# One program per engine for recurrence, branch and dense part; the guard in front of the last product; the second product three tiles behind

## The reference

```python
for t in range(S):
    y[:, :, t] = np.einsum('bhd,bhde->bhe', rt, state)
    Sa = np.einsum('bhde,bhe->bhd', state, at)
    state_decay = state * wt[:, :, None, :] - np.einsum('bhd,bhe->bhde', Sa, bt)
    state = state_decay + np.einsum('bhd,bhe->bhde', vt, kt)
...
h = x @ w_in                                   # 3072 x 320 by 320 x 2048
g = np.where(h >= 1, h, np.where(h <= -1, 0, (h + 1) ** 2 / 4))
x = g @ w_out                                  # 2048 x 320
...
h = np.maximum(np.maximum(x @ w1, x @ w2), x @ w3)   # 320 x 768 each
return h @ w_out                               # 768 x 320
```

## Time and profile before

| | us |
|---|---|
| median of 3 runs | 1055.07 (1054.64 to 1055.91) |
| the profiled execution | 1052.78 |
| its span in the trace | 1051.1 |
| TensorE busy | 962.9 (92% of the span) |
| VectorE, ACT, POOL busy | 506.8, 393.1, 456.5 |
| mean granted clock of TensorE | 0.97 of full |

### The profile page before, as it was taken

The page is one execution under the profiler, slowest core; times in us unless marked ns, Lnnn a source line. Parts: engine busy times, 40 slices in busy tenths (PEclk is TensorE's granted clock), DMA queues, the critical chain, the costliest instruction groups (busy, mean ns, idle before and its releaser), DMA issues.

```text
span 1051.1 us, 29793 instructions
## 1 busy us (share of the span) xinstructions
PE 962.9 (92%) x12330; PEld 807.1 (77%) x12330; DVE 506.8 (48%) x700; ACT 393.1 (37%) x719; POOL 456.5 (43%) x633
## 2 busy tenths in 40 slices
PE   6648999899998887899999999999999999999998
PEld 5436787788776776677888788878887888888887
DVE  8886666667552452696333323332333243324321
ACT  1214455455554563464233323332333133313321
POOL 3586786959688841242133213321332133123311
PEclk9957999999998899999999999999999999999999
DMA  5854667676645631462000100010001000100000
GB/s 84 142 108 89 119 104 133 102 139 107 128 81 116 116 72 28 135 181 68 1 26 1 31 1 26 0 30 0 25 0 30 0 25 0 30 0 26 0 1 26
DMA packets 242915, 61.27 MB, mean 58 GB/s; under 512 B 223728, under 2 KB 238832, under 8 KB 242800
## 3 DMA queue, kind: packets, MB, share of 16 engines
q1 hardware_dynamic: 147760, 44.86, 19.3%
q10 hardware_dynamic: 95040, 14.76, 8.6%
HBM read 44.89 MB, written 14.68 MB: 57 GB/s over the span
## 4 chain that ended last, share of the span: by engine, by line
issue 27%; PE 17%; POOL 10%; DVE 3%; ACT 1%; DMA 1%; POOLq 0%; DVEq 0%; ACTq 0%; SPq 0%
POOL hid_lo L1399 10%; PE ring L1212 8%; PE acc L1212 5%; PE ring L1222 3%; PE ring L1254 2%; DVE sq L1457 1%; PE acc L1276 1%; DVE clip L1451 1%; DMA raw<-in_moe_w_dram 1%; DVE wmax_lo L1425 1%; ACT sq L1361 0%; ACT hid_hi L1337 0%; POOLq L35 0%; DVE win_lo L1425 0%; DVE wout_lo L1417 0%
## 5 line engine op out<-in xcount | busy, mean ns | idle before, releaser
L1399 POOL TENSOR_TENSOR hid_lo<-sq,hid_hi 128x512 fp32r<-128x512 f32 x132 | 174.4, 1321 | 453.5 <-ACT hid_hi L1337 453.5
L1451 DVE TENSOR_SCALAR clip<-ring 128x512 f32<-128x512 f32 x96 | 66.2, 690 | 132.1 <-PE ring L1222 132.1
L448 POOL TENSOR_TENSOR prod<-sysX 128x30 f32<-128x30 f32 (+14 forms) x193 | 101.8, 527 | 58.1 <-DMA sysX<-systems 42.8
L1337 ACT CAST hid_hi<-sq 128x512 fp32r<-128x512 f32 x132 | 82.0, 622 | 93.5 <-DVE sq L1457 71.5
L1361 ACT ACTIVATE sq<-clip 128x512 f32<-128x512 f32 x96 | 60.7, 633 | 147.7 <-DVE clip L1451 145.9
L452 POOL TENSOR_TENSOR sysX<-sysX,prod 128x30 f32<-128x30 f32 (+14 forms) x193 | 106.9, 554 | 15.1
L1457 DVE SCALAR_TENSOR_TENSOR sq<-clip,sq 128x512 f32<-128x512 f32 x96 | 67.9, 708 | 59.9 <-ACT sq L1361 59.9
L1212 PE MATMUL acc<-hid_hi,wout_hi 128*128 128x512 f32 x192 | 76.4, 398 | 7.7 <-POOL hid_lo L1399 7.6
L1482 DVE TENSOR_TENSOR sq<-ring,clip 128x512 f32<-128x512 f32 x36 | 24.9, 692 | 120.4 <-PE ring L1222 98.1
L1383 ACT COPY clip<-ring 128x512 f32<-128x512 f32 x36 | 21.1, 587 | 153.8 <-PE ring L1222 153.8
L1212 PE MATMUL ring<-x_hi,win_hi 128*128 128x512 f32 x192 | 75.5, 393 | 3.4 <-PEq L958 3.4
(11 more groups left out here) (166 smaller groups left out, 2177.4 us busy)
## 6 DMA issues: line engine op xcount, KB each, us to landing
nat_k<-in_k_dram ACTq DMA_DIRECT2D x48, 80.0 KB, 3.4
vz<-in_v_dram SPq DMA_DIRECT2D x96, 40.0 KB
nat_r<-in_r_dram SPq DMA_DIRECT2D x96, 40.0 KB, 2.8
xT<-yT SPq DMA_DIRECT2D x96, 40.0 KB
out_dram<-res SPq DMA_DIRECT2D x24, 160.0 KB, 1.8
inverses_T<-sysX SPq DMA_DIRECT2D x7, 512.0 KB, 4.5
nat_w<-in_w_dram ACTq DMA_DIRECT2D x44, 80.0 KB
nat_a<-in_a_dram ACTq DMA_DIRECT2D x44, 80.0 KB, 3.5
```

The source lines that it names most:

```text
L448: g_.tensor_tensor(some, X[:, 0:j, j:j + 1].to_broadcast([P, j, rest]), X[:, j:j + 1, j + 1:BLK].to_broadcast([P, j, rest]), ALU.mult)\
L1337: nc.scalar.copy(hid[(u if u < T1 else u - T1) % HB][0][:, :], src).then_inc(hid_hi, 1)
L1399: nc.gpsimd.tensor_tensor(hid[at % HB][1][:, :], sq[at % 2][:, :], f32(hid[at % HB][0][:, :]), ALU.subtract)\
L1451: nc.vector.tensor_scalar(clip[f % 2][:, :], ring[(f + 2) % 4][:, :], -1.0, None, ALU.max).then_inc(clipped, 1)
```

## The change

Three things change.

1. The three parts become one block. Each engine has one program: recurrence, then branch, then dense part. No engine drains or meets the others between them. The semaphores of all parts live to the end. VectorE sets a new semaphore x_ready (with a memset of one element, `settled`) after the branch; TensorE waits for it before its first dense matmul. SP loads the weight pieces as soon as it is through the branch, and waits for y_stored only behind them.
2. The guard moves. Its checks stand in front of VectorE's last `rr`, its matmul in front of TensorE's last `xy` (into the bank of `w`), its compare and the load of the flag in front of VectorE's last `y`; SP loads the flag in front of its last y store.
3. In the first phase of each dense block the second product follows three tiles behind (AHEAD = 3). LAG stays 2 in the second phase, and HB stays 3.

```diff
             def store(g):
+                if g == NG - 1:
+                    sp.wait_ge(flag_step, 5)
+                    kept["flag"] = sp.value_load(unsafe[0:1, 0:1], min_val=0, max_val=1)
                 sp.wait_ge(out["y"], g + 1)
...
                 need(done["yt"], g + 1)
+                if g == NG - 1:
+                    other, at = latest[BANK["w"]]
+                    for reader in READERS.get(other, (other,)):
+                        need(out[reader], OUTS.get(reader, 1) * (at + 1))
+                    need(flag_step, 3)
+                    nc.tensor.matmul(bank_of["w"][0:1, 0, 0:1], fit[:, :], ones[:, :], start=True, stop=True)\
+                        .then_inc(flag_step, 1)
                 ps = bank_of["ys"]
...
-            pe.wait_ge(flag_step, 3)
-            nc.tensor.matmul(pair[0][0:1, 0, 0:1], fit[:, :], ones[:, :], start=True, stop=True)\
-                .then_inc(flag_step, 1)
...
+            def take_flag():
+
+                dve.wait_ge(flag_step, 4)
+                nc.vector.tensor_scalar(unsafe[:, :], bank_of["w"][0:1, 0, 0:1], P - 0.5, None, ALU.is_lt)\
+                    .then_inc(flag_step, 1)
+                dve.wait_ge(flag_step, 5)
+                kept["flag"] = dve.value_load(unsafe[0:1, 0:1], min_val=0, max_val=1)
+
             def rr(g):
+                if g == NG - 1:
+                    within_bounds()
...
             def y_(g):
+                if g == NG - 1:
+                    take_flag()
...
-            sp.wait_ge(y_stored, 64 * NG)
             for i in range(len(pieces)):
                 load_piece(i)
+            sp.wait_ge(y_stored, 64 * NG)
...
-                for f in range(LAG, T1 + LAG):
+                for f in range(LAG, T1 + AHEAD):
                     if f < T1:
                         hidden(n, f, first)
-                    u = f - LAG
+                    u = f - AHEAD
+                    if u < 0:
+                        continue
...
+            pe.wait_ge(x_ready, 1)
             blocks(pe, one_block)
...
+        @block.vector
+        def _(dve):
+            flag = recur_dve(dve)
+            again_dve(dve, flag)
+            nc.vector.memset(settled[:, :], 1.0).then_inc(x_ready, 1)
+            dense_dve(dve)
```

More of the change, by code:

```diff
@@ L215, in program @@
                 steps[n](at)
-        before, last = {}, {}
+        before, latest = {}, {}
         for n, g in sequence("PE"):
             if n not in OPENS and n not in MORE:
-                before[n, g] = last.get(BANK[n])
-                last[BANK[n]] = next((c for c, o in OPENS.items() if o == n), n), g
+                before[n, g] = latest.get(BANK[n])
+                latest[BANK[n]] = next((c for c, o in OPENS.items() if o == n), n), g
         raw = [rates[g % RATED][:, 0:PIECE] for g in (14, 15, 16)]
@@ L378, in _, with recur_pool @@
                     | {f"load {n}{j}": load(sp, n, j, 0) for n in ("r", "v") for j in range(2)})
-        @block.gpsimd
-        def _(pool):
+            return kept["flag"]
+        def recur_pool(pool):
             g_ = nc.gpsimd
@@ L998, in _, with again_dve @@
                 load_x(sp, x, xT, 0, x_again)
-        @block.vector
-        def _(dve):
-            flag = dve.value_load(unsafe[0:1, 0:1], min_val=0, max_val=1)
+        def again_dve(dve, flag):
             with dve.If(flag > 0):
@@ L1516, in build, with _ @@
         win = list(zip(win0, win1, win2))
-        attention(nc, w, a, b, k, r, v, xT, *scratch, unsafe, early, y_stored, x, x1, w_in, win)
-        step_by_step(nc, w, a, b, k, r, v, xT, unsafe, y_stored, x, x1)
-        dense(nc, xT, w_in, w_out, w1, w2, w3, w_last, y, y_stored, x, x1, win)
+        signals = ctx.enter_context(ExitStack())
+        x_ready = signals.enter_context(nc.semaphore("x_ready"))
+        recur_sp, recur_pe, recur_act, recur_dve, recur_pool = \
+            attention(nc, signals, w, a, b, k, r, v, xT, *scratch, unsafe, early, y_stored, x, x1, w_in, win)
+        again_sp, again_dve = step_by_step(nc, signals, w, a, b, k, r, v, xT, y_stored, x, x1)
+        dense_sp, dense_pe, dense_act, dense_dve, dense_pool = \
+            dense(nc, signals, xT, w_in, w_out, w1, w2, w3, w_last, y, y_stored, x_ready, x, x1, win)
+        block = ctx.enter_context(nc.Block())
+        @block.sync
+        def _(sp):
+            flag = recur_sp(sp)
+            again_sp(sp, flag)
+            dense_sp(sp)
+        @block.tensor
+        def _(pe):
+            recur_pe(pe)
+            dense_pe(pe)
+        @block.scalar
+        def _(act):
+            recur_act(act)
+            dense_act(act)
+        @block.gpsimd
+        def _(pool):
+            recur_pool(pool)
+            dense_pool(pool)
+        @block.vector
[4 more added lines that the diff above has]
+            dense_dve(dve)
 _INS = ["w", "a", "b", "k", "r", "v", "moe_w_in", "moe_w_out", "moe2_w1", "moe2_w2", "moe2_w3",
```

79 lines of the change are left out of this document (35 added, 44 removed).

## The result

The changed kernel takes 1042.4 us (median of 4 runs, 1041.22 to 1044.84) where the kernel before takes 1054.86 (4 runs, 1052.28 to 1055.91): a ratio of 0.99, with a 95% interval of 0.9879 to 0.992. That is 12.5 us by the medians, and 8.4 to 12.8 by the interval. The profiled execution took 1043.04 us with a span of 1041.3; before, 1052.78 and 1051.1. So the two profiled executions are 9.8 us apart.

The account below looks back on a forecast made before the run. TensorE was taken to bound blocks 1 to 5, VectorE block 0. Distance -4.8 and handover -3.2 gave -8.0 from 1052.78, so 1044.8, plus 2.3 to the median: 1047.0 us; own range 1045.8 to 1048.2, wider 1044.4 to 1050.6.

Parts of the forecast that it names:

- The distance: Blocks 1 to 5: second product three tiles behind removes TensorE's stall for hid_lo at five tile ends, 4.8 us.
- (c): Rival, ends of dense blocks: tile 15's hid_lo comes later with the same shift, gain only 3.2 us, 1051.9; chance 0.04.
- (d): Rival, blocks 1 to 5: hid_hi's wait for the product of tile f-3 holds ACT, slower, 1059; chance 0.03.
- The handover's path: Recurrence to dense part: guard covered, skip 0.6 us, TensorE starts at 421.2 to 421.8, 3.0 to 3.6 us earlier.
- Rival (a): Handover: dense part starts later through a fetched skip target or half clock, 3.2 us shrink to 1 to 2, 1048.6; chance 0.13.
- What the earlier start is worth: Block 0: first weight pieces start VectorE's chain earlier, and the full 3.2 us reach the block's end.
- (b): Rival, block 0: handover gives nothing at its end because contention or transfers set VectorE's pace, 1050.2; chance 0.06.
- (f): Rival: nothing gained from handover and hid_lo late too, all gains lost, 1055.1; chance 0.03.
- From there the chain runs as before: Block 0, from ACT's first weight split: split, hid_hi, split, square, then VectorE's gate of tile 1, afterwards saturated; shift 3.2 us.
- The half clock: First two hidden tiles of block 0: TensorE at half clock would cost 1.5 to 3 us, little counting; full clock taken.
- the median of the runs, 1055.07, lies 2.3 above it, which makes 1047.0: Whole kernel: the 2.3 us between profiled execution and median was added to the forecast 1044.8.
- half a microsecond each: Forecast's own range, 1045.8 to 1048.2: allowance for the skip, the landing and VectorE's pace.

Follow-up runs that it names:

- kernel 3: The kernel before, three blocks kept, with only the second product moved to three tiles behind: ratio 0.9943 to the kernel before.
- kernel 4: The changed kernel with the second product four tiles behind, still three hidden buffers: ratio 0.9885 to the kernel before.
- kernel 9: The changed kernel with POOL writing block 0's zeros and the guard's matmul in front of xy's wait for rr: 1041.4 us, ratio 0.989 to the kernel before.
- 1: The changed kernel again, no edit: 1042.23 us, ratio 0.9888 to the kernel before.
- 10: The changed kernel again, no edit, beside kernel 9 on one chip: 1042.37 us, ratio 0.9887 to the kernel before.
- 7: The changed kernel with block 0's five zero writes made by POOL instead of VectorE: 1037.88 us, ratio 0.9874 to the kernel before.
- 5: The changed kernel with SP loading the weight pieces only when y is stored: ratio 0.9935 to the kernel before.
- 2: The changed kernel with the second product back at two tiles behind: ratio 0.9946 to the kernel before.
- 6: The changed kernel, blocks still joined, with the guard and flag loads back behind the last product and y: ratio 0.9958 to the kernel before.
- 11: The kernel of 9 run again without edit: one run, 1040.8 us.

## Where the prediction was right, and which steps failed

**The distance: predicted 4.8, measured 5.1.** Behind p15 the changed kernel takes 621.2 - 64.85 = 556.4 us, the kernel before 631.2 - 69.76 = 561.4; kernel 3 alone gives the same. The stall of hid_lo is gone from blocks 1 to 5, and nothing came in its place, as predicted. The later blocks last 101.35 us (the first 101.5) for a predicted 101.4. Also as predicted, hid_hi's wait binds nowhere, which kernel 4 shows with far more of it, so (c) and (d) fall.

**The handover's path: right in its order, and its clock times partly by luck.** The load and compare are covered by rr and xy, the skip lies beside y, and then come the first dense matmul at 421.19 (421.2 to 421.8), the clip at 423.89 (423.8), the pieces at 422.94 (422.75). That these times agree to 0.2 us is luck: they hang on where the recurrence ends, and in the repeats the first dense matmul starts at 423.10 and 418.25. What the traces do show is the distance: the first dense matmul starts 2.8 us behind xy's first in all three, for a forecast of 2.9 to 3.5. Two small terms were off. The forecast let rr come 0.1 us late behind the guard's checks; rr stands at 417.00 for 416.89, but POOL's last total is 0.12 later too, and rr follows it by 0.58 for 0.59, so the checks cost nothing. And the guard's matmul, which I had "ready near 417.1", stands on TensorE behind the wait for rr and starts at 418.28, 0.12 us on the path, which kernel 9 gives back. Rival (a) needed a skip of up to 3.7 us or half clock. The skip took 0.6 us at most and the clock was 1.00. The Trainium skill (Runtime: NRT & Kernel Launch, section on instruction fetch mechanics) describes a wait for a page by DMA behind a branch to a target outside the window already fetched. This trace shows no such wait; whether the target lay outside the window, no run here shows.

**The first step that failed is the 3.2 us of "What the earlier start is worth".** It was put too small; it measured 4.5 to 4.9, and p15 comes at 484.95 for a forecast of 486.4. Measured from xy to p15, the changed kernel gains 69.76 - 64.85 = 4.9 us (4.5 to 4.6 in 1, 4 and 10). The owner was right: VectorE is the one that is full in block 0 (7), it is paced by its first pieces (5), and the third tile is worth nothing there (2, 3). So (b) and (f) fall: the handover is worth 4.4 us at the end of kernel 2. Two parts of the number were too small.

First, the start of the chain. I let the first pieces take 3.7 us to land, as in the earlier trace rows, which gave ACT's split at 426.45. They took 3.3 (3.2 in kernel 1), and the split began at 426.07, 3.13 us behind the issue: from xy it is 3.6 to 3.8 earlier, not 3.2. Both figures are medians of two transfers, and ACT's split waits for the first alone, which took 3.5 us before and 3.1 in the changed kernel; so 0.2 of the error was in the reading, and 0.4 in the transfer. VectorE's gate of tile 1 followed, 3.8 to 4.1 earlier. Why the same transfer is shorter was not tried. It isn't that it lies beside y's store: in kernel 5, where it is issued only when y has landed, it took 3.0 too, and in all kernels with joined programs 2.9 to 3.1, in kernel 3 3.4.

Second, "From there the chain runs as before". From gate to p15 it took 57.33 us before and 57.29 in kernel 3, but 56.44 in the changed kernel and 56.52 to 56.88 in 1, 2, 4, 5, 6 and 10: 0.4 to 0.9 less, in every kernel with joined programs and the zeros on VectorE, also where the handover is late (5, 6). VectorE's busy time in block 0 is lower by the same order (55.89 to 54.88). The two traces show where it lies. Counted from the gate of tile 1, VectorE's operations in the changed kernel are 0.27 us ahead right behind that gate (1.25 us for 0.98), 0.40 after 8 us, 0.89 after 32 us, and from there the two run alike. The last step is one operation of 1.95 us,

```profile
462.57 1.95 DVE L1425 TENSOR_TENSOR wmax_lo<-raw,wmax_hi 64x768 fp32r<-64x768 f32 x1
```

which takes 0.95 in the changed kernel, less 0.52 that the one before it takes longer there:

```profile
458.90 0.95 DVE L1437 TENSOR_TENSOR wmax_lo<-raw,wmax_hi 64x768 fp32r<-64x768 f32 x1
```

The long one began beside POOL's hid_lo, the short one behind it:

```profile
461.73 1.98 POOL L1399 TENSOR_TENSOR hid_lo<-sq,hid_hi 128x512 fp32r<-128x512 f32 x1 [2.18 <-ACT hid_hi L1337]
```

```profile
456.77 1.30 POOL L1412 TENSOR_TENSOR hid_lo<-sq,hid_hi 128x512 fp32r<-128x512 f32 x1 [1.41 <-ACT hid_hi L1351]
```

So these rows point to which of VectorE's operations lie beside one of POOL. It isn't the gate of tile 1 alone: in kernel 3 that took only 0.68 us, and the whole still 57.29. That POOL lengthens them is only argued from such rows; no run holds everything else and moves POOL's work alone. Why they fall better with joined programs stays open.

**The half clock was judged too lightly.** I wrote that it would cost 1.5 to 3 us of TensorE's time, "of which little counts". It didn't occur in the changed kernel, so it cost the forecast nothing, but kernel 6 shows it: when TensorE rests longer, the first clip waits for tile 0 at the lower level, and p15 comes 1.5 to 1.7 us later than I expected of it. Tile 0's matmuls take 1.34 us more; that these are most of it follows from the sum, no run shows it apart.

**The second step that failed is "the median of the runs, 1055.07, lies 2.3 above it, which makes 1047.0".** It carried the distance between one profiled execution and the median over to the new kernel as if it were fixed, and put the recurrence's own spread at nothing. Before, the median is 2.1 to 2.3 us above the profiled execution; in the changed kernel it is 0.6 below it (1042.4 for 1043.04). That is 2.9 of the 4.6 us by which the forecast missed; the other 1.7 are the dense part, less 0.24 us of later xy. With 10 in place of 8 the forecast would have been 1045.1, inside the range; the last 2.7 us are the medians against the profiled executions (12.5 for 9.8).

In twelve traces of kernels with joined programs xy starts between 415.06 and 425.58 us (mean 419.3), and in the two with three blocks at 419.36 and 419.86; single runs of the kernel before lie from 1048.21 to 1064.38. The three runs that I had were 1.3 us apart, and I took "half a microsecond each" for three terms of the dense part and nothing for this. By the traces the changed kernel gains 9.6 to 10.0 behind xy; by the three timings 10.5, 11.8 and 11.9. Each interval holds the traces' value, except that the third ends at 9.9. All 16 timed runs against all 64 of the kernel before give 11.3 us by the means, with a standard error of 0.5 (an estimate, since they come from several sets of runs). Whether the joined program also gains 1 to 2 us ahead of xy stays open: the timings lean that way, but they stray from the traces as far in kernels where this can't be the reason, 1.4 us more gain in kernel 3, which touches nothing ahead of the dense part, and 3.0 less in kernel 9.

## What to carry to other kernels

Where an engine is saturated in the first stretch behind a handover, ask what starts its chain: here the first weight pieces did, and a microsecond of theirs was a microsecond at the block's end, while more distance was worth nothing there. TensorE's own start counted as soon as it came later than they did (6). A greater distance between producer and consumer paid by about the stall at the phase's end (5.1 us for 4.8), and a ring that seems one too short may be waited for at length without cost, if the wait lies behind enough other work. Before a range is set, look for a stage that varies by itself: three runs within 1.3 us said nothing of one whose end spreads over 10.

## What the runs showed of the hardware that I had not expected

- After waits of 1.35 and 0.82 us TensorE's granted clock was still at 1.00 (changed kernel); after 1.10 and 1.90 us it was 0.50 over 422 to 424 us and 0.70 over the next two (kernel 6). The guard behind the last product made the dense part start 2.4 us later and its first tile 1.34 us longer; 2.6 us of it reached the end.
- A taken branch over some 80 instructions took 0.6 us before and at most 0.6 in the changed kernel, where it was hidden beside y: the memset behind it started at 421.07, as y (420.42 + 0.69) ended.
- Moving five zero writes from VectorE to POOL (memsets of 0.5 to 0.7 us each) shortened block 0 by 3.8 to 4.2 us of the 5.9 that VectorE was spared; its waits for ACT's square grew from 2.8 to 4.7 us.
- The recurrence ends up to 7.3 us apart in executions of one and the same kernel (415.06 and 422.34 in 9 and 11), with TensorE's granted clock at 0.95 and 0.92 on average up to there, and the dense part behind it repeats to 0.4.
